# Fused retention, expert layers and MLP on one core: loads paced by the landing of earlier ones, weight order shifted

## The reference

```python
# q, k, v: (2, 8, 576, 64); gamma per head; rel = i - j
scores = q @ k.T / sqrt(64)
ret = scores * where(rel >= 0, gamma ** rel, 0)
x = (ret @ v) as (1152 tokens, 512)
# four experts, w1: (4, 512, 1024), w2: (4, 1024, 512)
p = probs / (probs.sum(-1) + 1e-9)
x = sum over e of p[:, e] * (relu(x @ w1[e]) @ w2[e])
# MLP, w_in: (512, 2048), w_out: (2048, 512)
h = x @ w_in
out = (h * tanh(softplus(h))) @ w_out
```

## Time and profile before

| | |
|---|---|
| runs | 619.34, 621.52, 625.62 us; median 621.52 |
| profiled execution | 619.39 us, span 617.3 us |
| TensorE busy | 604.9 us (98%) |
| GpSimd, VectorE, ScalarE busy | 278.5, 265.1, 234.8 us |
| DMA moved | 50.47 MB, mean 82 GB/s; 345, 340 and 225 GB/s in the first three of 40 slices |

### The profile page before, as it was taken

One profiled execution on the slowest core, in us unless ns is written; L12 is line 12 of the kernel. 1 busy time (PEld: TensorE's weight loads), 2 busy tenths in 40 slices (PEclk: granted clock), 3 DMA queues, 4 the chain that ended last, 5 costly groups with the idle time before them and its releaser, 6 DMA issues.

```text
span 617.3 us, 9709 instructions
## 1 busy us (share of the span) xinstructions
PE 604.9 (98%) x3952; PEld 546.4 (89%) x3952; DVE 265.1 (43%) x365; ACT 234.8 (38%) x434; POOL 278.5 (45%) x230
## 2 busy tenths in 40 slices
PE   7799999999999999999999999999999999999997
PEld 5788999999899999999999999989989999989996
DVE  5477654323254433154434154535545432334334
ACT  2466244322233321323332223435455454334431
POOL 2668645534435535335554435532446543443300
PEclk9899999999999999999999999999999999999999
DMA  9963222322112332012331112321112232201002
GB/s 345 340 225 103 72 66 65 109 72 64 35 34 69 107 100 69 34 35 69 102 102 54 50 35 69 103 68 52 52 35 65 67 101 75 69 0 52 2 0 103
DMA packets 24923, 50.47 MB, mean 82 GB/s; under 512 B 2864, under 2 KB 2992, under 8 KB 24880
## 3 DMA queue, kind: packets, MB, share of 16 engines
q1 hardware_dynamic: 24736, 49.84, 25.2%
q10 hardware_dynamic: 144, 0.02, 0.0%
HBM read 47.49 MB, written 2.36 MB: 81 GB/s over the span
## 4 chain that ended last, share of the span: by engine, by line
PE 95%; DMA 2%; issue 1%; DVE 1%; SPq 1%; ACT 1%
PE bank L527 31%; PE bank L529 31%; PE bank L528 31%; DMA w_raw<-in_weights 2%; PE bank L651 1%; PE bank L459 1%; PE bank L489 1%; PE bank L493 1%; SPq L423 0%; DVE acc_sb L945 0%; DVE acc_sb L949 0%; PE bank L464 0%; SPq L420 0%; ACT st L728 0%; ACT xa_hi L734 0%
## 5 line engine op out<-in xcount | busy, mean ns | idle before, releaser
L412 POOL TENSOR_TENSOR w_lo<-w_raw,w_hi 128x512 fp32r<-128x512 f32 x96 | 134.4, 1414 | 147.8 <-ACT w_hi L385 144.3
L527 PE MATMUL bank<-w_hi,h_hi 128*128 128x512 f32 x432 | 168.7, 390 | 0.0
L529 PE MATMUL bank<-w_hi,h_lo 128*128 128x512 f32 x432 | 168.4, 390 | 0.0
L528 PE MATMUL bank<-w_lo,h_hi 128*128 128x512 f32 x432 | 168.3, 390 | 0.0
L932 DVE TENSOR_TENSOR h_act<-part,bank 128x384 f32<-128x384 f32 x96 | 52.9, 552 | 170.4 <-PE bank L529 169.9
L407 POOL TENSOR_TENSOR ws<-ws_f,ws 128x1024 fp32r<-128x1024 f32 x24 | 58.4, 2432 | 144.8 <-ACT ws L381 144.8
L529 PEld LDWEIGHTS bank<-w_hi,h_lo 128*128 128x128 f32 x432 | 81.1, 188 | 16.9
L528 PEld LDWEIGHTS bank<-w_lo,h_hi 128*128 128x128 f32 x432 | 81.1, 188 | 12.3
L527 PEld LDWEIGHTS bank<-w_hi,h_hi 128*128 128x128 f32 x432 | 81.0, 188 | 12.1
L764 ACT ACTIVATE part<-bank 128x384 f32<-128x384 f32 x72 | 35.4, 491 | 138.8 <-PE bank L529 138.8
L899 DVE SCALAR_TENSOR_TENSOR h_lo<-h_act,h_hi 128x384 fp32r<-128x384 f32 x64 | 73.3, 1155 | 20.9 <-ACT h_hi L754 20.3
(11 more groups left out here) (98 smaller groups left out, 867.6 us busy)
## 6 DMA issues: line engine op xcount, KB each, us to landing
w_raw<-in_weights SPq DMA_DIRECT2D x144, 256.0 KB, 2.7
loaded<-in_toks SPq DMA_DIRECT2D x9, 512.0 KB, 7.7
loaded<-in_feats SPq DMA_DIRECT2D x8, 512.0 KB, 7.0
out<-acc_sb SPq DMA_DIRECT2D x6, 256.0 KB, 2.1
out<-acc_sb SPq DMA_DIRECT2D x1, 768.0 KB, 3.5
loaded<-in_first SPq DMA_DIRECT2D x1, 726.0 KB, 4.5
ident<-in_ident SPq DMA_DIRECT2D x1, 64.0 KB, 4.7
p_nat<-in_probs ACTq DMA_DIRECT2D x1, 18.0 KB, 5.3
```

The lines of the kernel that those rows point to most:

```text
L412: pool.tensor_tensor(w_lo[layer][:, x], w_raw[:, r % RAW], w_hi[layer][:, x].bitcast(F32), ALU.subtract).then_inc(s_wl, 1)
L527: pe.matmul(out, w[0], x[0], start=first, stop=False, **more)
L528: pe.matmul(out, w[0], x[1], start=False, stop=False, **more)
L529: return pe.matmul(out, w[1], x[0], start=False, stop=last, **more)
```

## The change

The SP queue gets waits for landings: from chunk 4's features on, a load is issued only when the third one ahead of it has landed (features, tokens and weights counted together), with one weight ahead of chunk 4's features where there were two, and the later weights interleaved with features and tokens. This holds up to the eighteenth weight load (`PACED`); the identity matrix is loaded there and no longer right behind the tokens. The weight jobs stand one turn later, and the first sum job ("s", 0, 0) moves from turn 7 to turn 9, behind unit 3 of w2; units 4 and 5 of w2 come behind it and behind the turns (`IN_STAGE[0]`). On ScalarE the first job of turn 3 goes ahead of tile 0's relu, the sum job's high part behind the first x sum, units 4 to 7 behind the second. On GpSimd the turn's low parts go ahead of the decay of chunk c + 2.

```diff
--- before.py
+++ after.py
@@ -58,11 +58,11 @@
 
 TILE_AMID = {3: 0}
 TILES_IN = {3: (1,), 4: (2,), 5: (3,), 6: (4,), 7: (5, 6), 8: (7,)}
-JOBS_IN = {1: (("w1", 0, 0),), 2: (("w1", 0, 1), ("w1", 0, 2)), 3: (("w1", 0, 3),), 4: (("w1", 0, 4), ("w1", 0, 5)),
-           5: (("w1", 0, 6),), 6: (("w1", 0, 7), ("w2", 0, 0)), 7: (("w2", 0, 1), ("w2", 0, 2), ("s", 0, 0)),
-           8: (("w2", 0, 3), ("w2", 0, 4)), 9: (("w2", 0, 5),)}
-
-WEIGHTS_IN = (2, 2, 2, 2, 2)
+JOBS_IN = {2: (("w1", 0, 0),), 3: (("w1", 0, 1), ("w1", 0, 2)), 4: (("w1", 0, 3), ("w1", 0, 4)), 5: (("w1", 0, 5),),
+           6: (("w1", 0, 6),), 7: (("w1", 0, 7), ("w2", 0, 0)), 8: (("w2", 0, 1), ("w2", 0, 2)),
+           9: (("w2", 0, 3), ("s", 0, 0))}
+
+PACED = 18
 ROWS_IN = {4: 5, 5: 6, 6: 7, 7: 8}
 PROBS_IN = 5
 WARM_START, WARM_NEXT = 7, 5
@@ -133,6 +133,8 @@
     for turn, jobs in JOBS_IN.items():
         for job in jobs:
             add(IN_TURN, turn, *job)
+    add(IN_STAGE, 0, "w2", 0, 4)
+    add(IN_STAGE, 0, "w2", 0, 5)
     add(IN_STAGE, 1, "w2", 0, 6)
     add(IN_STAGE, 1, "w2", 0, 7)
     for s in range(2, ALL_STAGES):
@@ -429,21 +431,59 @@
                 sp.dma_start(w_raw[:, r % RAW], weights_in[2 * UNITS * e + UNITS * layer + u])\
                   .then_inc(s_raw[r % RAW], 16)
 
+            def feats_there(c):
+                sp.wait_ge(s_feats[c % SLOTS], landed(c))
+
+            def toks_there(c):
+                sp.wait_ge(s_toks[c % SLOTS], landed(c))
+
+            def weights_there(r):
+                sp.wait_ge(s_raw[r % RAW], 16 * (r // RAW + 1))
+
             sp.dma_start(loaded[:, lead - CONSTS:lead + 2 * KIND], first_in).then_inc(s_feats[0], 16)
             load_toks(0)
             for c in range(1, SLOTS):
                 load_feats(c)
                 load_toks(c)
-            at = 0
-            for c in range(SLOTS, PLACES):
-                for r in range(at, at + WEIGHTS_IN[c - SLOTS]):
-                    load_weights(r)
-                at += WEIGHTS_IN[c - SLOTS]
+            load_weights(0)
+            feats_there(SLOTS - 1)
+            sp.wait_ge(s_o, 1)
+            load_feats(SLOTS)
+            weights_there(0)
+            load_toks(SLOTS)
+            feats_there(SLOTS)
+            load_weights(1)
+            toks_there(SLOTS)
+            sp.wait_ge(s_o, 2)
+            load_feats(SLOTS + 1)
+            weights_there(1)
+            load_weights(2)
+            load_toks(SLOTS + 1)
+            feats_there(SLOTS + 1)
+            load_weights(3)
+            weights_there(2)
+            sp.wait_ge(s_o, 3)
+            load_feats(SLOTS + 2)
+            toks_there(SLOTS + 1)
+            load_weights(4)
+            weights_there(3)
+            load_toks(SLOTS + 2)
+            for c in range(SLOTS + 3, PLACES):
+                at = 2 * (c - SLOTS) - 1
+                feats_there(c - 1)
                 sp.wait_ge(s_o, c - SLOTS + 1)
                 load_feats(c)
+                weights_there(at - 1)
+                load_weights(at)
+                toks_there(c - 1)
                 load_toks(c)
-            sp.dma_start(ident[:, :], ident_in).then_inc(s_id, 16)
-            for r in range(at, len(LOADS)):
+                feats_there(c)
+                load_weights(at + 1)
+            for r in range(2 * (PLACES - SLOTS) - 1, len(LOADS)):
+                if r < PACED:
+                    weights_there(r - 3)
+                if r == PACED:
+                    sp.dma_start(ident[:, :], ident_in).then_inc(s_id, 16)
                 load_weights(r)
             by_rows = out.rearrange("(g p) d -> p g d", p=P)
             sp.wait_ge(s_af, read(EXPERTS - 1, TT - 1))
@@ -790,15 +830,22 @@
                 for job in IN_TURN.get(c - 1, ()):
                     if JOBS[job][0] == "s":
                         job_hi(act, job)
+                ahead = 1 if c in TILE_AMID else 0
+                for job in IN_TURN.get(c, ())[:ahead]:
+                    job_hi(act, job)
                 if c in TILE_AMID:
                     plain_hi(*divmod(TILE_AMID[c], ITEMS))
-                for job in IN_TURN.get(c, ()):
+                for job in IN_TURN.get(c, ())[ahead:]:
                     if JOBS[job][0] != "s":
                         job_hi(act, job)
             for n in range(4):
                 t_hi(0, n)
+                if n == 0:
+                    for job in IN_TURN[PLACES]:
+                        if JOBS[job][0] == "s":
+                            job_hi(act, job)
                 if n == 1:
-                    for job in IN_STAGE[1]:
+                    for job in IN_STAGE[0] + IN_STAGE[1]:
                         job_hi(act, job)
 
             for s in range(2, ALL_STAGES):
@@ -1098,10 +1145,12 @@
             v_decay(0)
             v_decay(1)
             for c in range(TURNS):
+                for job in IN_TURN.get(c, ()):
+                    job_lo(pool, job)
                 if c + 2 < PLACES:
                     v_decay(c + 2)
-                for job in IN_TURN.get(c, ()):
-                    job_lo(pool, job)
+            for job in IN_STAGE[0]:
+                job_lo(pool, job)
             pool.wait_ge(s_tl, 4)
             for s in range(1, ALL_STAGES):
                 for job in IN_STAGE.get(s, ()):
```

## The result

The changed kernel's median is 623.86 us over 21 runs, that of the kernel before 621.17 over its 21; the ratio is 1.0037, 95% interval 1.0019 to 1.0055. The range of the forecast ended at 622.8. A second comparison (10 runs) gave 1.0019 (0.9993 to 1.0046), which alone does not tell the change from none. The profiled execution took 623.59 us, span 621.5, against 619.39 and 617.3.

A forecast was written before the change was run, and what follows sets the result against it. TensorE, busy for 98% of the span, bounds the kernel, so time can only be won in retention. Terms 2.1 + 1.4 - 0.6 - 1.7 gain 1.2 us: 619.39 becomes 618.2, plus 1 for scatter 619.2; range 615.8 to 622.8.

The forecast's parts named there:

- Step 7: Behind tile 7: late sums delay w2 unit 4's low part; TensorE waits 0 to 3.1 us, 1.7 taken.
- Step 4: Tile 0 in turn 3: full clock expected if the hole shrinks, twelve matmuls 3.5 to 2.1 us, gain 1.4.
- Step 2: Turn 3: TensorE's instruction-fetch hole of 2.33 us at 18.85 becomes 0.75 (bounds 0 and 2.33), gain 1.58.
- the sign that the prediction set itself: Mechanism counts as wrong if turn 3's hole shrinks but tile 7 ends less than 1.5 us earlier.
- the rule that the prediction set against itself: DMA engines alternate between queue rows packet by packet, so turn 3's 2.33 us hole stays while they are full.
- rival C: Turn 3: hole stays at 2.33 us, clock falls, 0.2 gain left, 1.7 still lost; 621.9 us, chance 0.25.
- Step 3: Turn 2: without ScalarE's weight wait, tile 0 starts at 20.4; gain 2.1 us, one path with Step 2.
- Step 5: From turn 3 on: TensorE reaches instruction block ends sooner, so holes may grow; 0.6 us lost.
- Step 1: SP load queue: three loads open; chunk 8's features land at 35.5, wanted about 41.5; no cost, 6 us slack.
- Step 6: GpSimd within a turn: weight's low part ahead of value decay costs nothing; otherwise 1 us per turn at most.
- The scale: Whole kernel: profiled execution would become 618.2 us; median expected 1 above, 619.2, where no change is 620.4.

The follow-up runs named there:

- e2: The kernel before with only the late sums (unit 3, then the sum job, in turn 9), no pacing, no other shift; 1.0094.
- e7_again: Second profile of the changed kernel with 12 dummy matmuls of zeros ahead of the first product that needs unit 4; that kernel measured 1.0005.
- e4: The changed kernel without pacing and with the sums back in turn 7, leaving the weight jobs' shift and GpSimd's order; 1.0072 against the kernel before.
- e3: The changed kernel without the pacing, with shifted jobs, GpSimd's order and late sums kept; 1.0062 against the kernel before.
- e6: The changed kernel with w1 unit 7, w2 units 0 to 4 and the sum job moved to earlier turns; 1.0011 against the kernel before.
- e11: The kernel of e9 with GpSimd's four sums taken out of the sum job and put at the start of turn 8; 1.004 against the kernel before.
- e12: The kernel of e11 with the pacing ended after the ninth weight load instead of the eighteenth; 1.0029 against the kernel before.
- e1_again: Second profile of the changed kernel with the first weight sums back in turn 7; that kernel measured 1.0034 against the kernel before.
- e9: The changed kernel with w2 unit 3 in turn 8 and unit 4 ahead of the sum job in turn 9; 1.0027 against the kernel before.
- e10: The kernel of e9 with five dummy matmuls of zeros ahead of tile 0 in turn 3; 1.0015 against the kernel before.

## Why the prediction was wrong, step by step

- **Step 7 failed, by its size.** It was priced at 1.7, called the middle between 0 and 3.1 (that is 1.55); it is 2.94 of wait and 3.2 in all, in each of three profiles. The term that it had too small is the four sums: 5.1, where 3.0 to 4.2 was allowed, and unit 4's low part took 2.0 where 1.27 to 1.81 was; the low part of the sums came at its lower bound, 2.2. "VectorE is busy with x sums only in the first part of it" was the wrong half of the argument: it is busy in that part with just the operations that double GpSimd's, and the earlier trace rows had shown the stretch. The row nearest to the new place was the slow one. The statement that the cost does not depend on what was won before held. e2 shows the step by itself: late sums alone on the kernel before bring a wait of 3.12.
- **Step 4 failed as a certainty.** The forecast counted the full clock at tile 0 as won (1.4). It held in one profile of three. Where it held, retention took 43.1, 3.5 to 4.6 shorter than before, more than the 2.9 forecast; where it fell, 45.9 and 46.2. The matmuls ahead of tile 0 leave the clock to chance: it fell at 22.47 behind a wait of 1.32 and holes of 0.53 and 0.51, at 22.57 behind a hole of 1.24, and not behind a wait of 1.23 and a hole of 0.69. Of the timed executions 5 of 31 kept it, and those took 618.8 to 619.8. That this is the forecast's 619.2 is luck: more was won in retention and more lost in step 7.
- **Step 2 held against the profile it was made from.** No hole of over 2 us is left in turn 3 or elsewhere: the total of the holes without a releaser (those of 0.25 or more) in turns 1 to 8 is 4.9, 4.6 and 4.8 before and 3.1, 2.1 and 4.1 after. The largest hole is 0.8 to 1.6 in all twelve profiles with pacing, 2.2 to 2.7 in five of the six without, 1.3 in the sixth. But the hole of turn 3 was there in one of three profiles of the kernel before, and in the third of the changed kernel one of 1.24 stands in that turn, over the 0.75 forecast. By the sign that the prediction set itself (the hole shrinks but tile 7 ends less than 1.5 earlier) its mechanism failed in the first profile: tile 7 ends at 55.31 where it was 54.34, and counted from the scores of chunk 1 only 0.3 earlier.
- **What the holes are.** The DMA records bear out the reading as instruction blocks: of the 67 such holes in the 18 profiles, 66 end 1.2 to 1.6 us after the end of a 16 KB instruction packet. All but four of those packets took 0.9 to 1.1 us, at full DMA share (1.11, at 18.73, ahead of the end of the hole of 2.33) as at less. So a long hole is a packet that starts late, not one that moves slowly. In five of the six profiles without pacing the packet of the largest hole started at 30.7 to 32.0, within about 0.5 us of the moment when the load queue ran dry, which agrees with the backlog holding it; when it was asked for, no trace shows. By the rule that the prediction set against itself (rival C) the hole would have stayed. It did not, but the share of the DMA engines there fell too, from 1.0 to between 0.7 and 0.9, so backlog and share are not told apart.
- **Step 3 brought little.** ScalarE no longer waits for a weight in turn 2, but in two of three profiles of the kernel before it did not either. The low part took 1.37 instead of 0.69, so tile 0 began 2.6 behind the scores of turn 3, where 2.2 was forecast; before it was 4.0 in one profile and 2.6 in the others.
- **Step 5** came true against the profile it started from: the holes behind turn 3 sum up to 2.1, 1.4 and 2.1 (the largest 1.2 to 1.4), where that profile has 1.5: 0.6 lost in two of three. The other two of the kernel before have 2.7 and 3.4 there, so it is no loss against them.
- **Step 1 held, without its slack.** TensorE waited for features in none of the changed kernel's profiles behind turn 1, and they landed after 3.5 to 5.6 when paced. But those of chunk 8 landed at 39.7 to 40.7, where 35.5 was forecast: 4.4, 0.6 and 3.9 ahead of turn 7's scores instead of 6, and in e7_again, with the shortest retention, TensorE waited 0.36 for them. So little more can be won in retention with this pacing.
- **Step 6** cost nothing that a profile shows by itself, but on GpSimd everything is a turn later, and e4 shows the price of that, 4.5 us, which the forecast did not have as a term at all; pacing gives about half of it back.
- The scale: I placed the new median 1 below that of the runs shown, as scatter. With 21 runs the old median stayed at 621.2; the profile that the sum started from was one of the early starts (scores at 7.80), 1.4 to 1.6 better than the other two.

Rival C gave 621.9, nearest to the outcome, but for another reason than the one that came true.

## What to carry to other kernels

Price work that is moved onto an engine by the duration it has beside its new neighbours: here GpSimd's sums went from 0.75 to 1.42 us. Look at more than one profile before a forecast is built: here the hole, the late weight and the fallen clock of turn 3 stood together in one of three. When work moves later, add up all that then stands in the queue up to the deadline, and look at which of it is wanted first; reordering afterwards only moves the wait. And where TensorE idles, take the clock as a chance with two outcomes, and profile each kernel more than once before a difference of 1 us is explained.

## What was not expected of the hardware

- VectorE and GpSimd slow each other: a 128x256 sum on GpSimd takes 0.75 alone and 1.46 beside VectorE's 128x768 operations, and those take 0.95 alone and 1.5 to 2.0 beside GpSimd. The Trainium skill, page "GPSIMD Engine Reference", section 1 (Specifications), lists GpSimd's SBUF interfaces as shared with VectorE, with contention when VectorE's instruction reads two SBUF inputs. The trace agrees: the operations that double read two, and one with an operand in PSUM kept its 0.55 beside GpSimd.
- The first matmuls run at full or at half pace by chance (the five ahead of chunk 1's scores take 1.25 or 2.1 us), and all that follows stands 1.4 us earlier or later.
- A wait of TensorE behind tile 7 was followed by a fallen clock in e2, e3 and e4 (2.93 to 3.16), in e6 (2.09; 0.77 from 60 to 65), e11 (4.00; 0.55 from 60 to 65) and e12 (3.67; 0.75 from 55 to 60), and not in the changed kernel (2.94 three times), e1_again (1.97), e9 or e10 (2.6 at P6). So the length of the wait alone does not say whether the clock falls.
